# Tap products of blocks 1 and 2 summed by TensorE, halved weight low parts, and a new order of the opening

## Chip, cores and metric

The kernel runs on one core of one Trainium2 chip. The metric is device time in microseconds (us) from start to end of one execution, the median of several. An engine is named as the profile names it: PE is TensorE, DVE is VectorE, ACT is ScalarE, POOL is GpSimd, SP is SyncE, which issues most of the transfers.

## What is computed

A convolution whose taps come from the input, then two feed-forward layers, on 8192 tokens of 192 features (2 sequences of 4096):

```
w   = exp(weight_gen - max over 7 taps);  w = w / (sum over taps + 1e-9)          # 8 heads x 7 taps per token
x   = sum over k in 0..6 of w[:, k] * x_pad[token + k]                             # causal, one weight per head of 24 features
h   = x @ w_in                                                                     # 192 -> 2048
P   = a0 + a1 h + a2 h^2 + a3 h^3;   Q = 1 + |b0||h| + |b1| h^2;   g = P / (Q + 1e-6)
y   = g @ w_out                                                                    # 2048 -> 192
yn  = y / sqrt(mean(y^2) + 1e-6) * rms_g
out = (silu(yn @ w_gate) * (yn @ w_val)) @ w2_out                                  # 192 -> 1536 -> 192
```

## The kernel before

**Tiling.** The tokens are cut into 16 blocks of 512 (4 slots of 128). All weights stay in SBUF. Each product with w_in, w_gate and w_val is made of five matmuls on parts that are kept in a format with fewer bits: a high part, and a low part that holds the rest (`first_layer`). So each such weight has to be copied to its high part by ACT (`piece_high`) and its low part taken by a subtraction once at the start: pieces 0 to 3 (w_in) by DVE, pieces 4 to 7 (w_gate, w_val) by POOL, 128x1536 each (`piece_low`, L390). A piece is loaded into a buffer that is free at the start: piece 4 into `seed`, 5 and 6 into `stage`, 7 into `glu`.

**Stages of a block.** The 7 tap products and their 6 sums (rows by tokens); transposes of the sum on PE into two PSUM banks (`xpose`); high and low parts of the transposed x (`x_high` on ACT, `x_low` on DVE); 16 chunks of the first layer (`up1`, bank, five matmuls); for each chunk two ACT passes (`linear`) and three DVE passes (`horner`, L601, L602, L604, one operand in PSUM); per pair of chunks |Q| (`abs`), per four the reciprocal square root (`root`), its square (`square`), then on DVE `py` (L617), `qy` (L612) and `newton` (L623), all three with both operands in SBUF, 1024 columns; 16 `down1`; row norm (`ss`, `rms`, `xn`); its transposes (`xnx`), 12 `gate`, 12 `value`, `silu`, `glu` products, 12 `down2` into the banks of `dn2`, and the copy to the output (`y`).

**Order.** Each engine runs an order written out by hand (`PE_PROGRAM`, `ACT_PROGRAM`, `DVE_PROGRAM`, `POOL_PROGRAM`): entries are step, number and lag; in iteration i a step works on block i - lag. So iteration i of PE holds `up1` of block i-1, parts of `down1`, `gate` and `value` of block i-2, and `down2` of block i-3. In iterations 1 and 2 (written out, outside the loop) no block has come as far as `down2`. An engine takes its steps strictly in order; a step waits on semaphores for what it reads and for the buffer that it writes (`bank_read` with the table `BEFORE` for the four shared banks).

**Taps before.** Block 0: DVE makes the 7 products and 2 of the sums (`first_product`, `first_sum`) and PE flips and adds five tiles by matmuls with the identity that accumulate in the two banks of `xpose` (`flip_and_add`, L755 and L761). From block 1 on POOL makes 7 products (L409, L413) and 6 sums (L422, L424, L427), and PE only transposes the result (L693). Ahead of iteration 1 ACT does `exp`, the high parts of pieces 0 to 4 and then `x_high` of block 0; `root 0` of block 0 waits for the low part of piece 4, since it writes `seed`. SP issues block 0's rows, all eight pieces, w_out, and only then (after the last tap product of block 0) block 1's rows.

Of the kernel before, what the change touches and what calls it, by code (L numbers as in the profile page):

```python
# [129 lines left out]
def build(nc, x, weight_gen, w_in, w_out, a, b, w_gate, w_val, w2_out, rms_g, out):  # L130
# [17 lines left out]
    with ctx:  # L148
# [66 lines left out]
        tap0 = sem("tap0")  # L215
        sum0 = sem("sum0")
# [163 lines left out]
        def _(pool):  # L380
# [35 lines left out]
            def tap_add(blk, k):  # L416
                wait(pool, tap_ready, (blk - 1) * K + k + 1)
                if k > 1:
                    wait(pool, tap_sum, (blk - 1) * (K - 2) + k - 1)
# [3 lines left out]
                else:  # L423
                    pool.tensor_tensor(conv_twice, conv[:, :, DA:D], product[:, :, DA:D], ALU.add)\  # L424
                        .then_inc(twice_ready, 1)
                    wait(pool, twice_ready, blk)
                    pool.tensor_tensor(conv_rows, conv_rows, product, ALU.add).then_inc(conv_ready, 1)  # L427

            def rms_inverse(blk, _):
# [8 lines left out]
                                                "piece": piece_low}, LAST)  # L438

        @block.scalar  # L440
        def _(act):
# [42 lines left out]
            def root(blk, t):  # L484
# [172 lines left out]
        def _(pe):  # L657
# [4 lines left out]
            def bank_read(blk, name, n):  # L662

                i = blk + LAG[name, n]
                while True:
# [140 lines left out]
```

## Time and profile before

| | us |
|---|---|
| median of 3 runs | 1449.33 (1448.91 to 1449.6) |
| the profiled execution | 1448.36, of which the trace spans 1446.6 |
| busy in the span | PE 1381.6 (96%), DVE 1251.5 (87%), ACT 1070.6 (74%), POOL 461.6 (32%) |

The page cuts the span into 40 slices of 36 us; PE is at 9 tenths or more in all but the first four. Times below are us from the start of the span. In a row of the timeline the bracket is the idle time of the engine ahead of the instruction and what ended it. "PEclk" is the granted clock of PE as a share of its full speed: 1.0 is 2.4 GHz, 0.5 is 1.2 GHz.

### The profile page before, as it was taken

How to read it: one execution, taken by the hardware profiler on the slowest of the kernel's cores; microseconds unless marked ns; L12 is line 12 of the kernel's file. 1: busy time of each engine (PE TensorE's matmuls, PEld its weight loads, DVE VectorE, ACT ScalarE, POOL GpSimd, SP SyncE). 2: the span in 40 equal slices, each digit the busy share in tenths (PEclk: the TensorE clock that was granted, in tenths of full speed). 3: DMA queues.
4: the chain of work that ended last, by engine and by line, in shares of the span. 5: the costliest groups of instructions: out<-in, count | busy, mean ns of one | idle time of the engine just before them, and what ended most of it. 6: DMA issues, size and time to landing. Idle time of an engine off the chain costs nothing.

```text
span 1446.6 us, 20719 instructions
## 1 busy us (share of the span) xinstructions
PE 1381.6 (96%) x7192; PEld 1233.7 (85%) x7192; DVE 1251.5 (87%) x1519; ACT 1070.6 (74%) x1387; POOL 461.6 (32%) x283
## 2 busy tenths in 40 slices
PE   7566999999999999999999999999999999999999
PEld 6355889888898988889898888989888898988988
DVE  6999998989989898998989899898989989888621
ACT  4766877878887787878778787877878887777521
POOL 1846241434324143432414343142434314200000
PEclk9778999999999999999999999999999999999999
DMA  8200001000000100000010000001000000000000
GB/s 230 84 0 21 11 0 42 1 31 11 30 11 0 41 0 30 11 30 11 0 41 0 30 11 30 11 0 41 0 30 11 30 12 0 12 0 1 12 12 11
DMA packets 12515, 32.31 MB, mean 22 GB/s; under 512 B 1604, under 2 KB 7234, under 8 KB 12480
## 3 DMA queue, kind: packets, MB, share of 16 engines
q1 hardware_dynamic: 11744, 31.61, 6.8%
q8 instruction: 22, 0.36, 0.1%
q10 hardware_dynamic: 736, 0.23, 0.1%
q14 instruction: 13, 0.11, 0.0%
HBM read 25.55 MB, written 6.29 MB: 22 GB/s over the span
## 4 chain that ended last, share of the span: by engine, by line
PE 76%; DVE 11%; ACT 7%; issue 4%; DMA 1%; SPq 0%; ACTq 0%; POOL 0%; DVEq 0%; POOLq 0%
PE dn L686 32%; PE bank L677 9%; PE bank L678 8%; PE bank L679 8%; PE bank L680 8%; PE bank L681 8%; DVE den L612 4%; ACT seed L490 2%; PE bank L693 2%; DVE num L604 2%; DVE num L617 1%; DVE num L601 1%; DVE num L623 1%; ACT L490 1%; ACT seed L496 1%
## 5 line engine op out<-in xcount | busy, mean ns | idle before, releaser
L686 PE MATMUL dn<-dn_w,num 128*128 128x192 f32 x2048 | 380.2, 330 | 17.1 <-DVE num L623 10.0
L686 PEld LDWEIGHTS dn<-dn_w,num 128*128 128x128 f32 x2048 | 344.9, 193 | 24.2 <-DVE num L623 8.6
L475 ACT ACTIVATE den<-bank,coef 128x512 f32<-128x512 f32 x256 | 175.6, 686 | 180.6 <-PE bank L681 163.7
L686 PE MATMUL dn<-dn_w,glu 128*128 128x192 f32 x1536 | 280.9, 327 | 5.3 <-DVE glu L648 5.3
L686 PEld LDWEIGHTS dn<-dn_w,glu 128*128 128x128 f32 x1536 | 254.3, 190 | 13.2 <-DVE glu L648 9.2
L601 DVE TENSOR_TENSOR num<-num,bank 128x512 f32<-128x512 f32 x256 | 174.0, 680 | 65.3 <-ACT num L477 63.4
L617 DVE SCALAR_TENSOR_TENSOR num<-num,coef,seed 128x1024 f32<-128x1024 f32 x128 | 184.8, 1445 | 38.9 <-ACT seed L496 38.4
L477 ACT ACTIVATE num<-bank,coef 128x512 f32<-128x512 f32 x256 | 199.8, 781 | 0.0
L623 DVE SCALAR_TENSOR_TENSOR num<-den,num 128x1024 f32<-128x1024 f32 x128 | 194.5, 1521 | 0.0
L602 DVE SCALAR_TENSOR_TENSOR den<-den,coef,bank 128x512 f32<-128x512 f32 x256 | 189.1, 739 | 0.0
L604 DVE SCALAR_TENSOR_TENSOR num<-num,coef,bank 128x512 f32<-128x512 f32 x256 | 189.0, 738 | 0.0
L612 DVE SCALAR_TENSOR_TENSOR den<-den,seed 128x1024 f32<-128x1024 f32 x128 | 188.1, 1470 | 0.0
L648 DVE TENSOR_TENSOR glu<-glu,bank 128x512 f32<-128x512 f32 x192 | 130.5, 680 | 66.1 <-PE bank L681 64.8
L516 ACT ACTIVATE glu<-bank 128x512 f32<-128x512 f32 x192 | 113.2, 598 | 81.2 <-PE bank L681 76.2
L422 POOL TENSOR_TENSOR conv<-conv,prod 128x768 f32<-128x768 f32 x75 | 170.2, 2270 | 0.0
L677 PE MATMUL bank<-xn_ah,up_ah 128*128 128x512 f32 x384 | 163.0, 425 | 0.0
L482 ACT ACTIVATE den<-den 128x1024 f32<-128x1024 f32 x128 | 134.9, 1054 | 32.1 <-DVE num L604 32.1
L413 POOL TENSOR_TENSOR prod<-x_in,w_blk 128x768 f32<-128x768 f32 x84 | 154.5, 1846 | 4.4
L678 PE MATMUL bank<-xn_al,up_ah 128*128 128x512 f32 x384 | 150.1, 391 | 0.0
L679 PE MATMUL bank<-xn_ah,up_al 128*128 128x512 f32 x384 | 149.9, 390 | 0.0
L680 PE MATMUL bank<-xn_b,up_bh 128*128 128x512 f32 x384 | 149.7, 390 | 0.0
L681 PE MATMUL bank<-xn_b,up_bl 128*128 128x512 f32 x384 | 149.5, 389 | 0.0
(106 smaller groups left out, 2004.5 us busy)
## 6 DMA issues: line engine op xcount, KB each, us to landing
x_in<-in_x_dram SPq DMA_DIRECT2D x14, 960.0 KB
out_dram<-y_out SPq DMA_DIRECT2D x16, 384.0 KB, 2.3
w_blk<-in_weight_gen_dram SPq DMA_DIRECT2D x14, 112.0 KB, 2.0
dn_w<-in_moe_w_out_dram SPq DMA_DIRECT2D x1, 1536.0 KB, 21.0
dn_w<-in_moe_w_out_dram SPq DMA_DIRECT2D x1, 1152.0 KB, 10.2
num<-in_moe_w_in_dram SPq DMA_DIRECT2D x1, 768.0 KB, 6.1
num<-in_moe_w_in_dram SPq DMA_DIRECT2D x2, 384.0 KB, 7.8
seed<-in_moe_w_gate_dram SPq DMA_DIRECT2D x1, 768.0 KB, 10.2
```

The source lines that it names most:

```text
L477: act.activation(chunk(num, c), h, ACT.Identity, scale=na(3), bias=na(2)).then_inc(lin_ready, 1)
L602: dve.scalar_tensor_tensor(d, d, B_ABS[:, 0:1], h, ALU.add, ALU.mult)
L604: dve.scalar_tensor_tensor(n, n, na(1), h, ALU.add, ALU.mult).then_inc(poly_ready, 1)
L612: dve.scalar_tensor_tensor(d, d, EPS_Q, y, ALU.add, ALU.mult).then_inc(qy_ready, 1)
L617: dve.scalar_tensor_tensor(n, n, na(0), y, ALU.add, ALU.mult).then_inc(py_ready, 1)
L623: dve.scalar_tensor_tensor(n, d, -2.0, n, ALU.add, ALU.mult).then_inc(act_ready, 1)
L677: pe.matmul(out_bank[:, :], ah, m_ah[:, :], start=True, stop=False)
L678: pe.matmul(out_bank[:, :], ah, m_al[:, :], start=False, stop=False)
L679: pe.matmul(out_bank[:, :], al, m_ah[:, :], start=False, stop=False)
L680: pe.matmul(out_bank[:, :], bh, m_b[:, :], start=False, stop=False)
L681: return pe.matmul(out_bank[:, :], bl, m_b[:, :], start=False, stop=True)
L686: done = pe.matmul(banks[:, j // 2, j % 2 * D:(j % 2 + 1) * D], acts[:, j * P:(j + 1) * P], w, start=first and j % 2 == 0, stop=last, skip ...
```

## The change

Iteration 1 holds the front of block 0 and the taps of block 1; iteration 2 those of blocks 1 and 2.

- For blocks 1 and 2 POOL makes the 7 products only, each into one of four tiles in turn. PE flips each product and adds it up in the two banks of `dn2`, which hold nothing before iteration 3 (steps `tap1` and `tap2`, placed in PE's order behind named `up1` and `down1` steps). The sums on POOL and the transposes of these blocks go. A product that reuses a tile waits until PE has flipped what was in it (`flipped`).
- The low parts of pieces 4 to 7 are taken in halves of 768 columns, eight instructions, each behind a DVE count (`LOW_BEHIND`); the products of block 2 are placed in the same way (`MUL_BEHIND`).
- Opening: ACT copies x of block 0 ahead of the high parts of pieces 3 and 4; pieces 4 to 7 go behind `abs 3`, `root 1`, `linear 9` and `abs 4`. SP loads block 1's rows ahead of w_out and of pieces 4 to 7. Piece 4 is staged in the buffer of `xn_t` and `square` in place of `seed`. DVE makes three of block 0's sums, PE flips four tiles.
- The rest follows from these (counts of semaphores that start at block 3, three guarding waits).

```diff
-down1 10 2, down2 1 3, down1 11 2, down2 2 3, value 3 3, gate 5 3, up1 4 1, value 4 3, up1 5 1, down1 12 2,
-down2 3 3, down1 13 2, value 5 3, up1 6 1, gate 6 3, up1 7 1, down2 4 3, down1 14 2, down2 5 3, down1 15 2,
-value 6 3, gate 7 3, value 7 3, gate 8 3, up1 8 1, up1 9 1, gate 9 3, up1 10 1, down2 6 3, down1 0 1,
+down1 10 2, down2 1 3, down1 11 2, down2 2 3, value 3 3, gate 5 3, up1 4 1, tap1 0 0, value 4 3, up1 5 1,
+tap1 1 0, down1 12 2, down2 3 3, down1 13 2, value 5 3, up1 6 1, tap1 2 0, tap2 0 0, gate 6 3, up1 7 1, tap1 3 0,
+tap2 1 0, down2 4 3, down1 14 2, down2 5 3, down1 15 2,
+value 6 3, gate 7 3, value 7 3, gate 8 3, up1 8 1, tap1 4 0, tap2 2 0, up1 9 1, tap1 5 0, tap2 3 0, gate 9 3,
+up1 10 1, tap1 6 0, tap2 4 0, down2 6 3, down1 0 1,
...
-down1 1 1, xnx 0 2, down2 9 3, down1 2 1, xnx 1 2, down1 3 1, up1 12 1, up1 13 1, up1 14 1, up1 15 1,
+down1 1 1, xnx 0 2, down2 9 3, down1 2 1, xnx 1 2, down1 3 1, tap2 5 0, up1 12 1, up1 13 1, tap2 6 0, up1 14 1, up1 15 1,
...
-silu 6 3, abs 2 1, linear 7 1, piece 5 1, ss 0 2, silu 7 3, abs 3 1, piece 6 1, silu 8 3, root 1 1, piece 7 1, linear 8 1, linear 9 1,
-linear 10 1, square 2 1, silu 9 3, abs 4 1, silu 10 3, linear 11 1, silu 11 3, square 3 1, xn_high 0 2,
+silu 6 3, abs 2 1, linear 7 1, ss 0 2, silu 7 3, abs 3 1, piece 4 1, silu 8 3, root 1 1, piece 5 1, linear 8 1, linear 9 1,
+piece 6 1, linear 10 1, square 2 1, silu 9 3, abs 4 1, piece 7 1, silu 10 3, linear 11 1, silu 11 3, square 3 1, xn_high 0 2,
...
-add 6 1, piece 5 2, piece 6 2, piece 7 2, less 0 0, norm 0 0, mul 0 0, mul 1 0, mul 2 0, add 1 0, mul 3 0, add 2 0, mul 4 0, rms 0 2, add 3 0,
-mul 5 0, add 4 0, mul 6 0, add 5 0,
+add 6 1, low 4 2, low 5 2, low 6 2, low 7 2, less 0 0, norm 0 0, mul 0 0, mul 1 0, mul 2 0, add 1 0, mul 3 0, add 2 0, mul 4 0, rms 0 2, add 3 0,
+mul 5 0, add 4 0, mul 6 0, add 5 0, low 0 1, low 1 1, low 2 1, low 3 1,
...
+ALONE = {"tap1": 1, "tap2": 2}
+FLIPPED_IN_SUMS = (0, 1, 2)
...
-              "mul": 1, "add": 1, "xpose": 1, "x_high": 1, "x_low": 1}
+              "mul": 1, "add": 3, "xpose": 3, "x_high": 1, "x_low": 1}
...
+            elif name in ALONE:
+                there = isinstance(i, int) and i - lag == ALONE[name]
...
-        xn_t = sb("xn_t", [P, SLOTS, D + DB])
+        norm_rows = sb("norm_rows", [P, SLOTS * (D + DB) + ROW])
+        xn_t = norm_rows[:, 0:SLOTS * (D + DB)].rearrange("p (j d) -> p j d", j=SLOTS)
+        square = norm_rows[:, SLOTS * (D + DB):].rearrange("p (j d) -> p j d", j=SLOTS)
...
-            ([w_gate[0:DA, :]], seed[:, 0:F2], up2_ah[:, 0, :], up2_al[:, 0, :]),
+            ([w_gate[0:DA, :]], norm_rows[:, 0:F2], up2_ah[:, 0, :], up2_al[:, 0, :]),
...
-        LOWS = len(PIECES) - BY_DVE
+        LOWS = 2 * (len(PIECES) - BY_DVE)
...
+        TILES = [slots(prod[:, 0, :]), slots(prod[:, 1, :]), conv_rows, y_out[:, :, :]]
+
+        def tile(blk, k):
+            return TILES[((blk - 1) * K + k) % len(TILES)]
...
+        def x_bank(blk, part):
+
+            if isinstance(blk, int) and blk in (1, 2):
+                return dn2[:, part, :]
+            return bank[XPOSE_BANK[part]][:, :]
...
-            for n in range(len(PIECES)):
+            for n in range(BY_DVE):
                 load_piece(n)
+            sp.wait_ge(tap0, K)
+            load_first(1)
             src, dst = DOWN[0]
             sp.dma_start(dst[:, :, :], src).then_inc(down_in[0], 16)
-            sp.wait_ge(tap0, K)
-            load_first(1)
             sp.dma_start(w_blk[:, :], w_rows[:, 2 * SLOTS * HK:3 * SLOTS * HK]).then_inc(wgen_in, 16)
+            sp.wait_ge(xt_ready, 2)
+            for n in range(BY_DVE, len(PIECES)):
+                load_piece(n)
             src, dst = DOWN[1]
             sp.dma_start(dst[:, :, :], src).then_inc(down_in[1], 16)
...
-            def piece_low(_, n):
-                pool.wait_ge(whi, n + 1)
-                pool.tensor_tensor(PIECES[n][3], PIECES[n][1], PIECES[n][2], ALU.subtract).then_inc(wlo, 1)
...
+            LOW_BEHIND = [(act_ready, 2)] * 3 + [(qy_ready, 3), (py_ready, 4)] + [(act_ready, 4)] * 3
+            MUL_BEHIND = [(qy_ready, 7)] * 3 + [(py_ready, 8)] * 2 + [(qy_ready, 9)] * 2
+
+            def half_low(_, n):
+                piece = BY_DVE + n // 2
+                cols = slice(n % 2 * F2 // 2, (n % 2 + 1) * F2 // 2)
+                pool.wait_ge(whi, piece + 1)
+                pool.wait_ge(*LOW_BEHIND[n])
+                pool.tensor_tensor(PIECES[piece][3][:, cols], PIECES[piece][1][:, cols], PIECES[piece][2][:, cols],
+                                   ALU.subtract).then_inc(wlo, 1)
...
-            pool.wait_ge(wlo0, BY_DVE)
-            piece_low(0, BY_DVE)
+
+            def early_product(blk, k):
+
+                turn = (blk - 1) * K + k - len(TILES)
+                if turn < 0:
+                    pool.wait_ge(xt_ready, 2)
+                elif turn % K == K - 1:
+                    pool.wait_ge(xt_ready, 2 * (turn // K + 2))
+                else:
+                    pool.wait_ge(flipped, turn // K * (K - 1) + turn % K + 1)
+                if k == 0:
+                    pool.wait_ge(x_in_ready, x_count(blk))
+                    pool.wait_ge(sm_norm, soft_count(blk))
+                if blk == 2:
+                    pool.wait_ge(*MUL_BEHIND[k])
+                pool.tensor_tensor(by_slot(tile(blk, k)), slot_heads(rows_of(k)), slot_heads(taps_of(k, blk)), ALU.mult)\
+                    .then_inc(tap_ready, 1)
...
-                if k == 0:
+                if isinstance(blk, int) and blk in FLIPPED_IN_SUMS:
+                    early_product(blk, k)
...
             exponentials(0, 0)
-            for n in range(5):
+            for n in range(3):
                 piece_high(0, n)
             x_high(0, 0)
             x_high(0, 1)
+            piece_high(0, 3)
...
-                if isinstance(blk, int) and (blk, t) == (0, 0):
-                    act.wait_ge(wlo, 1)
...
+                if isinstance(blk, int) and blk == 0:
+                    act.wait_ge(wlo, 2)
...
+                if isinstance(blk, int) and blk == 0:
+                    act.wait_ge(xt_ready, 6)
...
+                    dve.wait_ge(sum0, 2)
...
-            for k in range(5):
+            first_product(0)
+            for k in (1, 3, 5):
                 first_product(k)
-            first_sum(3)
-            for k in range(5, K):
-                first_product(k)
-            first_sum(5)
+                first_product(k + 1)
+                first_sum(k)
             for n in range(2):
...
+                        pe.wait_ge(x_ready, 6)
...
-            def flip_and_add(tile, first, last):
+            def flip_and_add(blk, rows, first, last):
                 for j in range(SLOTS):
-                    done = pe.matmul(bank[XPOSE_BANK[0]][:, j * P:(j + 1) * P], tile[:, j, 0:DA], ident[:, :],
+                    done = pe.matmul(x_bank(blk, 0)[:, j * P:(j + 1) * P], rows[:, j, 0:DA], ident[:, :],
                                      start=first and j == 0, stop=last, skip_group_check=True)
                 if last:
                     done.then_inc(xt_ready, 1)
                 for j in range(SLOTS):
                     for half in range(0, P, DB):
-                        done = pe.matmul(bank[XPOSE_BANK[1]][half:half + DB, j * P:(j + 1) * P], tile[:, j, DA:D], ident[:, :],
+                        done = pe.matmul(x_bank(blk, 1)[half:half + DB, j * P:(j + 1) * P], rows[:, j, DA:D], ident[:, :],
                                          start=first and j == 0, stop=last, skip_group_check=True)
                 if last:
                     done.then_inc(xt_ready, 1)
+                elif blk > 0:
+                    done.then_inc(flipped, 1)
+
+            def early_tap(blk, k):
+                pe.wait_ge(tap_ready, (blk - 1) * K + k + 1)
+                if (blk, k) == (2, 0):
+                    pe.wait_ge(x_ready, 4)
+                flip_and_add(blk, tile(blk, k), k == 0, k == K - 1)
             pe.wait_ge(consts, 3)
             for n in range(WARM):
                 pe.matmul(bank[XPOSE_BANK[0]][:, 0:P], ident[:, :], ident[:, :], start=True, stop=True)
-            for k in (0, 1, 2):
-                pe.wait_ge(tap0, k + 1)
-                flip_and_add(FIRST[k], k == 0, False)
-            pe.wait_ge(sum0, 1)
-            flip_and_add(FIRST[3], False, False)
-            pe.wait_ge(sum0, 2)
-            flip_and_add(FIRST[5], False, True)
+            pe.wait_ge(tap0, 1)
```

## Rows read from the trace of the kernel before

**Rows 1.** Stretches: length; busy PE, PEld, DVE, ACT, POOL; PEclk, DMA share, GB/s.

```profile
70.00:80.00 10.00, 3.82 (x11) 3.07 (x12) 10.00 (x6) 2.36 (x4) 10.00 (x3) 0.66 0.00 0
...
200.00:400.00 200.00, 199.10 (x1040) 178.22 (x1039) 181.51 (x223) 157.99 (x211) 73.17 (x45) 1.00 0.06 21
```

**Rows 2.** Chain that ended last, in order of time: start, length, what.

```profile
12.71 10.24 DMA seed<-in_moe_w_gate_dram
22.97 1.48 ACT up_ah L457
...
25.76 0.71 DVE x_b L576
26.56 0.76 PE bank L677
```

**Rows 3.** Timeline, block 0's flips on PE (start, us, engine, line, what).

```profile
18.86 1.16 PE L755 MATMUL bank<-ident,xn_t 128*128 128x128 f32 x8
19.95 1.09 PE L761 MATMUL bank<-ident,xn_t 128*64 128x128 f32 x16
```

**Rows 4.** Groups of DVE's instructions from 43 to 83 us: busy, mean ns.

```profile
L612 DVE SCALAR_TENSOR_TENSOR den<-den,seed 128x1024 f32<-128x1024 f32 x4 | 13.9, 3478 | 0.0
L623 DVE SCALAR_TENSOR_TENSOR num<-den,num 128x1024 f32<-128x1024 f32 x3 | 7.9, 2653 | 0.0
L617 DVE SCALAR_TENSOR_TENSOR num<-num,coef,seed 128x1024 f32<-128x1024 f32 x4 | 7.6, 1922 | 1.7 <-ACT seed L496 1.7
```

**Rows 5.** Timeline of DVE, opening and iterations 1 and 2.

```profile
9.39 1.83 DVE L564 TENSOR_TENSOR prod<-x_in,w_first 128x768 f32<-128x768 f32 x2 [0.68 <-DMA x_in<-in_x_dram]
...
43.95 4.94 DVE L617 SCALAR_TENSOR_TENSOR num<-num,coef,seed 128x1024 f32<-128x1024 f32 x2 [1.70 <-ACT seed L496]
...
74.13 0.68 DVE L601 TENSOR_TENSOR num<-num,bank 128x512 f32<-128x512 f32 x1
...
76.05 2.56 DVE L623 SCALAR_TENSOR_TENSOR num<-den,num 128x1024 f32<-128x1024 f32 x1
...
82.96 1.27 DVE L617 SCALAR_TENSOR_TENSOR num<-num,coef,seed 128x1024 f32<-128x1024 f32 x1
...
117.44 1.21 DVE L612 SCALAR_TENSOR_TENSOR den<-den,seed 128x1024 f32<-128x1024 f32 x1
```

**Rows 6.** Groups of DVE's instructions from 83.1 to 154.1 us.

```profile
L623 DVE SCALAR_TENSOR_TENSOR num<-den,num 128x1024 f32<-128x1024 f32 x8 | 13.4, 1690 | 0.0
L617 DVE SCALAR_TENSOR_TENSOR num<-num,coef,seed 128x1024 f32<-128x1024 f32 x9 | 12.1, 1352 | 0.7 <-ACT seed L496 0.7
L612 DVE SCALAR_TENSOR_TENSOR den<-den,seed 128x1024 f32<-128x1024 f32 x8 | 12.0, 1510 | 0.0
```

**Rows 7.** Timeline of POOL.

```profile
30.00 3.51 POOL L390 TENSOR_TENSOR up_al<-seed,up_ah 128x1536 fp32r<-128x1536 f32 x1 [12.97 <-DVE up_bl L550]
40.51 1.55 POOL L409 TENSOR_TENSOR conv<-x_in,w_first 128x768 f32<-128x768 f32 x1 [7.00 <-DMA x_in<-in_x_dram]
...
77.49 4.46 POOL L390 TENSOR_TENSOR up_bl<-glu,up_bh 128x1536 fp32r<-128x1536 f32 x1
```

**Rows 8.** Timeline of ACT.

```profile
57.63 2.00 ACT L490 ACTIVATE seed<-den,coef 128x2048 f32<-128x2048 f32 x1
...
60.91 0.67 ACT L475 ACTIVATE den<-bank,coef 128x512 f32<-128x512 f32 x1
...
62.14 0.69 ACT L475 ACTIVATE den<-bank,coef 128x512 f32<-128x512 f32 x1
```

**Rows 9.** Timeline of PE: a wait in iteration 2, and `up1 14`.

```profile
117.58 5.49 PE L686 MATMUL dn<-dn_w,num 128*128 128x192 f32 x16 [4.46 <-DVE num L623]
...
154.94 0.50 PE L677 MATMUL bank<-x_ah,up_ah 128*128 128x512 f32 x1 [2.33 <-DVE xn_al L639]
```

**Rows 10.** Busy time by stretch, iteration 2, and one stretch at half clock.

```profile
103.60:154.90 51.30, 35.03 (x156) 29.87 (x154) 50.60 (x55) 35.58 (x52) 27.62 (x16) 0.87 0.07 22
117.50:123.00 5.50, 5.42 (x17) 5.42 (x18) 5.50 (x9) 5.35 (x6) 0.00 (x0) 0.50 0.00 0
```

More of the change, by code:

```diff
@@ L93 @@
 STORE_LAG = 2
-ONCE = ("piece",)
+ONCE = ("piece", "low")
+ALONE = {"tap1": 1, "tap2": 2}
+FLIPPED_IN_SUMS = (0, 1, 2)
 FROM_BLOCK = {"peak": 2, "less": 2, "exp": 2, "inverse": 2, "norm": 2,
-              "mul": 1, "add": 1, "xpose": 1, "x_high": 1, "x_low": 1}
+              "mul": 1, "add": 3, "xpose": 3, "x_high": 1, "x_low": 1}
 LAG = {(name, n): lag for name, n, lag in PE_PROGRAM}
 def run_iterations(eng, order, ops, last):
-    trail = max(lag for _, _, lag in order)
+    trail = max(3, max(lag for _, _, lag in order))
     def iteration(i):
@@ L215, in build @@
         tap0 = sem("tap0")
+        flipped = sem("flipped")
         sum0 = sem("sum0")
@@ L399, in _ @@
             pool.memset(x_in[:, 0:(HALO - SLOTS) * D], 0.0).then_inc(halo0, 1)
-            pool.wait_ge(wlo0, BY_DVE)
-            piece_low(0, BY_DVE)
+            def early_product(blk, k):
[13 more added lines that the diff above has]
+                    .then_inc(tap_ready, 1)
             def tap_product(blk, k):
-                if k == 0:
+                if isinstance(blk, int) and blk in FLIPPED_IN_SUMS:
+                    early_product(blk, k)
+                elif k == 0:
                     wait(pool, x_in_ready, x_count(blk))
@@ L411, in tap_product @@
                     if k >= 3:
-                        wait(pool, tap_sum, (blk - 1) * (K - 2) + k - 2)
+                        wait(pool, tap_sum, (blk - 3) * (K - 2) + k - 2)
                     pool.tensor_tensor(by_head(prod[:, k % 2, :]), rows_of(k), taps_of(k, blk), ALU.mult)\
@@ L418, in tap_add @@
                 if k > 1:
-                    wait(pool, tap_sum, (blk - 1) * (K - 2) + k - 1)
+                    wait(pool, tap_sum, (blk - 3) * (K - 2) + k - 1)
                 product = slots(prod[:, k % 2, :])
@@ L425, in tap_add @@
                         .then_inc(twice_ready, 1)
-                    wait(pool, twice_ready, blk)
+                    wait(pool, twice_ready, blk - 2)
                     pool.tensor_tensor(conv_rows, conv_rows, product, ALU.add).then_inc(conv_ready, 1)
@@ L437, in _ @@
                                                 "less": peak_taken_off, "norm": normalised_taps,
-                                                "piece": piece_low}, LAST)
+                                                "low": half_low}, LAST)
         @block.scalar
@@ L461, in x_high @@
                 wait(act, xt_ready, blk * 2 + (part + 1))
-                act.activation((x_ah, x_b)[part][:, :], bank[XPOSE_BANK[part]][:, :], ACT.Copy).then_inc(xt_hi, 1)
+                act.activation((x_ah, x_b)[part][:, :], x_bank(blk, part), ACT.Copy).then_inc(xt_hi, 1)
             exponentials(0, 0)
-            for n in range(5):
+            for n in range(3):
                 piece_high(0, n)
@@ L562, in first_product @@
                 elif k == 6:
-                    dve.wait_ge(sum0, 1)
+                    dve.wait_ge(sum0, 2)
                 dve.tensor_tensor(by_slot(FIRST[k]), slot_heads(rows_of(k)), slot_heads(taps_of(k, 0)), ALU.mult)\
@@ L573, in x_low @@
                 if part == 0:
-                    dve.tensor_tensor(x_al[:, :], bank[XPOSE_BANK[0]][:, :], x_ah[:, :], ALU.subtract).then_inc(x_ready, 1)
+                    dve.tensor_tensor(x_al[:, :], x_bank(blk, 0), x_ah[:, :], ALU.subtract).then_inc(x_ready, 1)
                 else:
-                    dve.tensor_tensor(x_b[DB:P, :], bank[XPOSE_BANK[1]][DB:P, :], x_b[DB:P, :], ALU.subtract)\
+                    dve.tensor_tensor(x_b[DB:P, :], x_bank(blk, 1)[DB:P, :], x_b[DB:P, :], ALU.subtract)\
                        .then_inc(x_ready, 1)
-            for k in range(5):
+            first_product(0)
+            for k in (1, 3, 5):
                 first_product(k)
-            first_sum(3)
-            for k in range(5, K):
-                first_product(k)
-            first_sum(5)
+                first_product(k + 1)
+                first_sum(k)
             for n in range(2):
@@ L668, in bank_read @@
                     blk = i - LAG[name, n]
-                    if not isinstance(blk, int) or 0 <= blk <= LAST or i < 0:
+                    if not isinstance(blk, int) or i < 0:
+                        break
+                    if 0 <= blk <= LAST and not (name == "xpose" and blk in (1, 2)):
                         break
@@ L696, in transposes @@
             def transposes(blk, part):
-                wait(pe, conv_ready, blk)
+                wait(pe, conv_ready, blk - 2)
                 bank_read(blk, "xpose", part)
@@ L768, in _ @@
                 pe.matmul(bank[XPOSE_BANK[0]][:, 0:P], ident[:, :], ident[:, :], start=True, stop=True)
-            for k in (0, 1, 2):
-                pe.wait_ge(tap0, k + 1)
-                flip_and_add(FIRST[k], k == 0, False)
-            pe.wait_ge(sum0, 1)
-            flip_and_add(FIRST[3], False, False)
-            pe.wait_ge(sum0, 2)
-            flip_and_add(FIRST[5], False, True)
+            pe.wait_ge(tap0, 1)
+            flip_and_add(0, FIRST[0], True, False)
+            for k in (1, 3, 5):
+                pe.wait_ge(sum0, (k + 1) // 2)
+                flip_and_add(0, FIRST[k], False, k == 5)
             pe.wait_ge(wlo0, 2)
@@ L779, in _ @@
                 "up1": up1, "down1": down1, "gate": gate, "value": value, "down2": down2,
-                "xnx": xn_transposes, "xpose": transposes}, LAST)
+                "xnx": xn_transposes, "xpose": transposes, "tap1": early_tap, "tap2": early_tap}, LAST)
 _INS = ['x', 'weight_gen', 'moe_w_in', 'moe_w_out', 'moe_a', 'moe_b',
```

1 line of the change is left out of this document (removed).

## Prediction

> **What bounds the kernel now.** The share of busy time names PE, but the stretches show two regimes. From 200 us on PE is busy 199.1 of 200 us at full clock [rows 1]: what is left there is a fixed amount of PE's work, and the change doesn't touch it. From about 26 to 155 us it is otherwise: between 70 and 80 us DVE and POOL are busy 10.0 of 10 us and PE 3.8 [rows 1]. The time is therefore set by how soon PE gets into its steady run. I date that by `up1 14` of block 1 at 154.94, PE's last wait ahead of it (2.33 us, for `xn_low` on DVE) [rows 9]; earlier by x, the whole is shorter by x.
>
> DVE's groups say why the opening is long. Before 83 us its passes with both operands in SBUF take 3.48, 2.65 and 1.92 us (L612, L623, L617) [rows 4], where the same passes take 1.21 and 1.27 us with POOL quiet [rows 5]. Passes with an operand in PSUM aren't stretched: a chunk's three passes ran from 74.13 to 76.05, 1.92 us, in a stretch in which POOL was never idle [rows 1, 5]. Against 1.21 (L612, L623) and 1.27 (L617) the excess up to 83 us is 13.9-4.8 + 7.9-3.6 + 7.6-5.1 = 15.9 us [rows 4]; after it 13.4-9.7 + 12.1-11.4 + 12.0-9.7 = 6.7 us [rows 6]. Together 22.6 us of DVE's path are owed to POOL.
>
> **1. The opening: 4.3 us.** The chain is x of block 0 [rows 2]: ACT's copy of x stood behind the high part of piece 4 (22.97 + 1.48), which waited for its load; the first matmul came at 26.56. Now the copy waits for the flips alone. DVE starts at 9.39 and makes one sum more: ten passes of 0.9 us [rows 5] end at 18.5; PE flips one tile less. A set is 18.86 to 21.04, 2.1 us start to start [rows 3]; the last set starts at 18.6 and ends at 20.8. Then ACT's copy of the second half (0.6 after 20.9), DVE's part of 0.71 and 0.1 to the matmul [rows 2]: 22.3. Gain 26.56 - 22.3 = 4.3. Piece 3's parts, now behind the copy, are ready at about 25.6, and `up1 4` needs them at 29. The 0.8 us that ACT, DVE and PE leave each other here is all known; bounds 3.5 to 4.6.
>
> **2. Iteration 1: 9.9 us.** Block 1's rows are issued at 17.5 and not behind six other transfers. They landed at 40.5 [rows 7]. Nothing shows their new time; piece 4, of the same size and also behind 2 MB, took 10.24 us [rows 2], so 27.7 at the latest and 17.5 as a floor. POOL's first product (1.55 us [rows 7]) is then ready by 29.3; PE asks for it at 30.2, behind `up1 4` (22.3 plus the 7.9 us that its first five `up1` took). Cover 0.9 us.
>
> PE has room for the seven sets (3.8 us busy of 10 at 70 us [rows 1]), but two stand in ACT's way. The first comes between `up1 4` and `up1 5` and holds `linear 5`, `abs 1` and `root 0` back by 0.7 us: `py 0`, at 43.95 before [rows 5], starts at 43.95 - 4.3 + 0.7 = 40.3. From there to `py 3` (82.96) DVE took 39.0 us, 23.1 without the excess of 15.9. Now the pieces' low parts wait until DVE reads PSUM. A half is 1.75 (half of 3.51) to 2.2 us (half of 4.46) [rows 7]; three of them (5.3 us) lie beside three chunks (5.8 us), the others beside one chunk each. Six of the products are over before 40 us; the seventh waits for the third set, at 39.4, and meets `py 0`: 0.8 us, between 0 and its whole 1.55.
>
> **A new wait** eats part of this. Once `newton` isn't stretched, ACT is late: behind `qy 1` come `root 1` (2.0 us), piece 5 (1.45 as in [rows 2]) and `linear 8` (1.23) [rows 8] before DVE may start `horner 8`. By hand along the queues: `qy 1` ends 49.65, but ACT is in piece 4 until 51.05; root until 53.05, piece until 54.5, linear until 55.75. DVE is through both newtons at 51.95: it idles 3.8 us. Pieces 6 and 7 delay `linear 10` and `11` for another 0.65 in sum. So 23.1 + 0.8 + 3.8 + 0.7 = 28.4 in place of 39.0, and `py 3` starts at 68.75, earlier by 14.2 (4.3 - 0.7 + 10.6; the 9.9 above).
>
> **3. Iteration 2: 3.5 us.** Up to `horner 0` of block 1 (102.6) POOL was quiet in both; the 14.2 stands. The products of block 2 now wait for `qy 6`, which gives back the 2.0 us that `py 6` and `qy 6` lost: 16.2. From here PE is the tighter queue. From 103.6 to 154.9 it was busy 35.0 of 51.3 us at a mean clock of 0.87; in 117.5 to 123.0 it ran at 1.2 GHz (0.50) after a wait of 4.46 us [rows 9, 10]. Without that stretch (2.7 us) and two shorter ones (1.6) its work is 30.7; seven sets of 2.1 make 45.4 us, and DVE needs 51.3 - 6.7 = 44.6 for its own. Two queues of 45 us that wait on each other don't both run full. By hand: waits of 2.5 us before `down1 12` (for `newton 6`) and 1.7 before `up1 6`; product 4 waits for a set that PE makes only behind `up1 6`, so it meets `newton 7` or `py 0`, and products 5 and 6, behind `rms`, meet `qy 1` and the newtons: 3.1 us for the three, between 0 and 3 x 1.55 = 4.7. `xn_low` then ends at 137.0 and PE reaches `up1 14` at 137.2: 154.9 - 137.2 = 17.7 us earlier. Four transposes go as well, but at that point PE and DVE are level, so I count nothing for them (up to 1 us).
>
> The other waits cost nothing: `y` of block 0 for the flips of block 2, `ss` for piece 4's low part and the first `down2` for `x_low` of block 2 all ask for what `up1 0` of block 2 or an earlier step had to have. SP's later pieces are wanted from 49.6 us on, 9 us after the whole load had ended before (the rows of block 1, behind w_out, landed at 40.5 [rows 7]).
>
> **Sum.** 4.3 + 9.9 + 3.5 = 17.7 us. Against the profiled execution, 1448.36 - 17.7 = 1430.7; the median of the runs lies 0.97 above that execution: 1431.6, and I give 1431.5.
>
> **A rule against the price of a meeting.** My 0.8 and 3.1 us let DVE and POOL both crawl on: two `py` took 4.94 where 2.5 are usual [rows 5]. The Trainium skill (SBUF — State Buffer, Who interferes with whom) says that the pair of ports is an exclusive lock: who comes first keeps it for the whole instruction. By it each of the four meetings costs DVE a product's whole length, 6.2 us in place of 3.9. This is in the second rival, and what hangs on the rule alone is 2.3 us.
>
> **Rivals.**
> *More of it (10%):* ACT gives nothing back, since pieces 4 and 5 lie better than by hand, and nothing meets: 3.8 + 0.7 less in iteration 1, of which PE passes on some 3 us: 21 us, 1427 to 1428. For it: the 22.6 are real. Against it: the order of ACT's steps is fixed and its durations are known.
> *More given back (28%):* meetings at the full length (+2.3), two or three PE waits of over 4 us that bring 1.2 GHz again (2.7 each [rows 10]), or rows of block 1 landing late by 2 us. Gain 9 to 14: 1435 to 1440. For it: in iteration 2 the loop product, set, tile, product is closed over three engines.
> *Not at all what it says (3%):* rows of block 1 still land at 40.5. Then PE waits for the first product behind `up1 4` until 42.1, `py 0` slips 12 us and the gain is 2 to 8 us: 1441 to 1447.
> *Slower (6%):* the sets don't fill gaps but stand in series. Each holds the next `up1`, so `linear`, `horner` and the product that asks for the tile. In series they cost 14 x 2.1 = 29.7, with ACT's 4.5 and the meetings' 3.9 38.1, against 22.6 + 4.3 = 26.9 saved: 11 us slower, 1460. It decides from about nine of the 14 sets in series (18.5 us). Against it: PE idled 6.2 of 10 us at 70 us and 16.3 of 51.3 later [rows 1, 10], and by hand one set of the first seven holds anybody up. A mild form, ten to eleven sets, gives 1451 to 1454.
>
> **How the numbers follow.** My forecast of 1431.5 with its own range of 1428 to 1435 has 53%. The range for 8 in 10 leaves out the slower case, the late rows and the tails of the others: 1426 to 1440. A measurement of this kernel tells about 0.2% (2.9 us) from no change. Faster by more: 53 + 10 + 28 and most of the 3, 0.92; within 0.2%: 0.03; slower by more: 0.05.
>
> **What would show each step.** Step 1: the first L677 at 22.3. Step 2: a DVE wait of about 3.8 us ahead of L601 for ACT's L477 near 52 us, `py 3` near 68.8, L612 at a mean near 1.3 before it, POOL's halves at 1.8 us. Step 3: PE busy over 90% from 89 us on, `up1 14` near 137. I am wrong if PE waits for POOL's products, if L612 and L623 still stretch beyond 1.6 us in the mean, or if after 140 us PE, now 18 us ahead, waits for DVE again.

## The result and the profile after

Four runs of the changed kernel gave a median of 1429.13 us (1427.42 to 1430.10) against 1449.12 of before (four runs, 1448.85 to 1449.60): 20.0 us less, ratio 0.986 with a 95% interval of 0.9843 to 0.9878. The profiled execution, the slowest of the four, took 1430.10, its trace spans 1428.3 us.

Busy time by stretch of the changed kernel (length; busy PE, PEld, DVE, ACT, POOL with their instructions; granted clock, DMA share, GB/s):

```profile
29.90:33.70 3.80, 3.80 (x27) 3.31 (x25) 3.80 (x7) 2.31 (x3) 1.19 (x1) 0.56 1.04 244
46.00:105.00 59.00, 45.06 (x241) 38.91 (x237) 54.16 (x71) 46.60 (x55) 22.57 (x14) 0.86 0.00 1
105.20:138.00 32.80, 32.74 (x264) 28.89 (x264) 32.74 (x41) 24.52 (x37) 8.96 (x5) 1.00 0.10 34
...
200.00:400.00 200.00, 199.10 (x1051) 178.95 (x1050) 179.86 (x225) 156.99 (x203) 63.37 (x40) 1.00 0.07 23
```

The last row is as before [rows 1]; the third is new: from 105.2 us on PE doesn't wait, where before it was busy 35.0 of 51.3 us [rows 10]. The groups of DVE from 43 to 69 us, which answer to [rows 4]:

```profile
L668 DVE SCALAR_TENSOR_TENSOR num<-num,coef,seed 128x1024 f32<-128x1024 f32 x4 | 5.0, 1281 | 3.4 <-ACT seed L544 3.4
L663 DVE SCALAR_TENSOR_TENSOR den<-den,seed 128x1024 f32<-128x1024 f32 x4 | 4.9, 1219 | 0.0
...
L652 DVE TENSOR_TENSOR num<-num,bank 128x512 f32<-128x512 f32 x6 | 4.1, 684 | 3.8 <-ACT num L527 3.8
L674 DVE SCALAR_TENSOR_TENSOR num<-den,num 128x1024 f32<-128x1024 f32 x3 | 3.6, 1220 | 0.0
```

`qy` (L663) takes 1.22 us in the mean where it took 3.48. In exchange DVE now waits 3.8 us in sum for ACT's `linear` (L527), 3.60 of them at 56.35. The dates of DVE on its path, from its timeline:

```profile
21.18 0.69 DVE L628 TENSOR_TENSOR x_b<-bank,x_b 64x512 fp32r<-64x512 f32 x1 [0.27 <-ACT x_b L511]
...
23.58 3.10 DVE L602 TENSOR_TENSOR up_bl<-num,up_bh 128x1536 fp32r<-128x1536 f32 x1
...
41.90 2.48 DVE L668 SCALAR_TENSOR_TENSOR num<-num,coef,seed 128x1024 f32<-128x1024 f32 x2 [3.35 <-ACT seed L544]
...
56.35 0.69 DVE L652 TENSOR_TENSOR num<-num,bank 128x512 f32<-128x512 f32 x1 [3.60 <-ACT num L527]
...
68.93 1.28 DVE L668 SCALAR_TENSOR_TENSOR num<-num,coef,seed 128x1024 f32<-128x1024 f32 x1
...
108.17 3.77 DVE L668 SCALAR_TENSOR_TENSOR num<-num,coef,seed 128x1024 f32<-128x1024 f32 x2
...
117.96 2.35 DVE L674 SCALAR_TENSOR_TENSOR num<-den,num 128x1024 f32<-128x1024 f32 x2
```

And of PE, with the first `up1`, the first two sets of flips and `up1 14` of block 1 (the last row):

```profile
21.98 0.47 PE L730 MATMUL bank<-x_ah,up_ah 128*128 128x512 f32 x1 [1.47 <-DVE x_b L628]
...
28.87 0.47 PE L730 MATMUL bank<-x_ah,up_ah 128*128 128x512 f32 x1 [2.07 <-DVE num L655]
...
30.32 1.91 PE L809 MATMUL dn<-ident,prod 128*128 128x128 f32 x8
32.16 1.59 PE L815 MATMUL dn<-ident,prod 128*64 128x128 f32 x16
...
34.96 1.05 PE L809 MATMUL dn<-ident,prod 128*128 128x128 f32 x8
35.94 1.09 PE L815 MATMUL dn<-ident,prod 128*64 128x128 f32 x16
...
66.79 0.79 PE L730 MATMUL bank<-x_ah,up_ah 128*128 128x512 f32 x1 [4.99 <-DVE num L655]
...
105.26 0.50 PE L730 MATMUL bank<-x_ah,up_ah 128*128 128x512 f32 x1 [1.38 <-DVE num L655]
...
138.02 0.50 PE L730 MATMUL bank<-x_ah,up_ah 128*128 128x512 f32 x1
```

`up1 14` came at 154.94 [rows 9] and comes at 138.02, 16.9 us earlier; the rest of the span shrank from 1291.7 to 1290.3 us. 16.9 + 1.4 = 18.3 us, the difference of the two spans.

### The profile page after: what moved, and what is told of

Same layout as the page of the kernel before. It is cut to its first block, busy times and chain, and to the rows that moved or that the text cites. A ratio compares the mean times of both kernels' runs of the same rounds, so it can differ in the third digit from the quotient of the medians.

```text
span 1428.3 us, 21289 instructions
## 1 busy us (share of the span) xinstructions
PE 1396.2 (98%) x7488; PEld 1249.2 (87%) x7488; DVE 1231.4 (86%) x1520; ACT 1070.5 (75%) x1387; POOL 430.9 (30%) x273
## 4 chain that ended last, share of the span: by engine, by line
PE 80%; DVE 8%; ACT 7%; issue 4%; DMA 0%; ACTq 0%; DVEq 0%
PE dn L739 34%; PE bank L730 9%; PE bank L731 9%; PE bank L732 9%; PE bank L734 9%; PE bank L733 9%; DVE den L663 3%; ACT seed L538 2%; PE bank L746 2%; ACT L538 1%; DVE num L655 1%; ACT seed L544 1%; ACT L502 1%; DVE num L652 1%; ACT num L527 1%
## 5 line engine op out<-in xcount | busy, mean ns | idle before, releaser
L739 PE MATMUL dn<-dn_w,num 128*128 128x192 f32 x2048 | 375.6, 328 | 4.0 <-DVE num L674 4.0
L739 PEld LDWEIGHTS dn<-dn_w,num 128*128 128x128 f32 x2048 | 340.9, 191 | 10.7 <-DVE num L674 5.2
L668 DVE SCALAR_TENSOR_TENSOR num<-num,coef,seed 128x1024 f32<-128x1024 f32 x128 | 181.7, 1421 | 43.0 <-ACT seed L544 42.5
L527 ACT ACTIVATE num<-bank,coef 128x512 f32<-128x512 f32 x256 | 199.9, 781 | 0.0
L674 DVE SCALAR_TENSOR_TENSOR num<-den,num 128x1024 f32<-128x1024 f32 x128 | 186.7, 1460 | 0.0
L663 DVE SCALAR_TENSOR_TENSOR den<-den,seed 128x1024 f32<-128x1024 f32 x128 | 176.9, 1383 | 0.0
L532 ACT ACTIVATE den<-den 128x1024 f32<-128x1024 f32 x128 | 134.9, 1055 | 19.3 <-DVE num L655 19.3
L471 POOL TENSOR_TENSOR conv<-conv,prod 128x768 f32<-128x768 f32 x65 | 147.2, 2264 | 0.0
L462 POOL TENSOR_TENSOR prod<-x_in,w_blk 128x768 f32<-128x768 f32 x78 | 142.5, 1834 | 4.1
```

What stands on the lines that cost most here:

```text
L527: act.activation(chunk(num, c), h, ACT.Identity, scale=na(3), bias=na(2)).then_inc(lin_ready, 1)
L663: dve.scalar_tensor_tensor(d, d, EPS_Q, y, ALU.add, ALU.mult).then_inc(qy_ready, 1)
L674: dve.scalar_tensor_tensor(n, d, -2.0, n, ALU.add, ALU.mult).then_inc(act_ready, 1)
L739: done = pe.matmul(banks[:, j // 2, j % 2 * D:(j % 2 + 1) * D], acts[:, j * P:(j + 1) * P], w, start=first and j % 2 == 0, stop=last, skip ...
```

## The experiments

Three groups of kernels, each beside runs of the kernel before of its own. "Gain" is the median of those minus the median of the kernel; the changed kernel has 20.0 and, run again in the second group, 20.2 us (ratio 0.9857, 0.9842 to 0.9872). A difference of two kernels under some 1 us isn't told apart by these runs. Below, a pass of DVE *meets* an instruction of POOL when the two run at once and the pass has both operands in SBUF, and its *excess* is what it takes beyond the 1.21 or 1.27 us (1.75 for a low part) that it takes with POOL quiet.

### The opening alone

```diff
 # before.py
-            for n in range(5):
+            for n in range(3):
                 piece_high(0, n)
             x_high(0, 0)
             x_high(0, 1)
+            piece_high(0, 3)
+            piece_high(0, 4)
...
 # and three first_sums on DVE, four flips on PE, as in the change
```

> The kernel before with one part of the change: ACT copies x of block 0 ahead of the high parts of pieces 3 and 4, DVE makes three sums, PE flips four tiles. SP's order, POOL's work and the staging stay. If the opening's 4.6 us (first up1 at 26.56 before, 21.98 after) is passed on whole to the end, 4.3 to 4.6 us less than before: 1444.6. If it is eaten later, because POOL's lows and sums meet DVE in other places, the gain is under 2 us.

Gain 10.0 us (1439.01 against 1448.98; ratio 0.9935, 0.9916 to 0.9954). Both readings were wrong: it gives twice what it takes off the opening. DVE's groups from 36 to 156 us, first of the kernel before, then of this one:

```profile
L612 DVE SCALAR_TENSOR_TENSOR den<-den,seed 128x1024 f32<-128x1024 f32 x12 | 25.9, 2166 | 0.0
L623 DVE SCALAR_TENSOR_TENSOR num<-den,num 128x1024 f32<-128x1024 f32 x11 | 21.3, 1953 | 0.0
L617 DVE SCALAR_TENSOR_TENSOR num<-num,coef,seed 128x1024 f32<-128x1024 f32 x12 | 18.4, 1549 | 2.4 <-ACT seed L496 2.4
```

```profile
L624 DVE SCALAR_TENSOR_TENSOR num<-den,num 128x1024 f32<-128x1024 f32 x12 | 22.5, 1890 | 0.0
L613 DVE SCALAR_TENSOR_TENSOR den<-den,seed 128x1024 f32<-128x1024 f32 x12 | 20.9, 1749 | 0.0
L618 DVE SCALAR_TENSOR_TENSOR num<-num,coef,seed 128x1024 f32<-128x1024 f32 x13 | 19.5, 1510 | 2.5 <-ACT seed L498 2.4
```

Against 1.21 and 1.27 us undisturbed [rows 5] the excess is 11.4 + 8.0 + 3.2 = 22.6 us before and 8.0 + 6.4 + 3.0 = 17.4 here. `py 0` starts at 38.61 (43.95 before), 5.3 us earlier; 5.3 + 5.2 = 10.5. POOL's work is the same, and its products still start at 40.3, when block 1's rows land; moved by 5 us against it, DVE's passes meet less of it (17.4 against 22.6). Nothing else of their work differs, so which passes are met is a matter of phase, and the parts of this change don't add up.

### Sums back on POOL

```diff
 # after.py
-FLIPPED_IN_SUMS = (0, 1, 2)
+FLIPPED_IN_SUMS = (0,)
-ALONE = {"tap1": 1, "tap2": 2}
+ALONE = {"tap1": -1, "tap2": -1}
-              "mul": 1, "add": 3, "xpose": 3, "x_high": 1, "x_low": 1}
+              "mul": 1, "add": 1, "xpose": 1, "x_high": 1, "x_low": 1}
...
 # the counts of tap_sum, twice_ready and conv_ready as before, x in the two shared banks
```

> The changed kernel with products and sums of blocks 1 and 2 back on POOL and transposes on PE; opening, placed halves of the low parts and ACT's order stay. Theory: sums on POOL meet DVE's passes in SBUF again, about 3 us in iteration 1 and the 6.7 us of before in iteration 2, less 2 us since no set of flips holds linear 5: 6 to 8 us slower than the changed kernel, 12 to 14 us faster than before, so 1435 to 1437. Rival, that the flips carry nearly the whole gain: 1443 or more. Rival, that PE's added work costs what POOL's sums cost: within 3 us of the changed kernel.

Gain 10.4 us (1438.56), 9.6 less than the changed kernel; I had expected 6 to 8 less. In the same window:

```profile
L661 DVE SCALAR_TENSOR_TENSOR den<-den,seed 128x1024 f32<-128x1024 f32 x12 | 20.1, 1680 | 0.0
L672 DVE SCALAR_TENSOR_TENSOR num<-den,num 128x1024 f32<-128x1024 f32 x12 | 18.6, 1566 | 0.0
L666 DVE SCALAR_TENSOR_TENSOR num<-num,coef,seed 128x1024 f32<-128x1024 f32 x12 | 18.6, 1559 | 2.4 <-ACT seed L542 2.4
```

The excess is 5.6 + 4.1 + 3.4 = 13.1 us; in the changed kernel it is 1.3 (one pair of `py`). `py 0` is 4.2 us earlier than before, the excess 9.5 us smaller, and DVE waits 3.6 us for ACT as in the changed kernel: 4.2 + 9.5 - 3.6 = 10.1. So the placed halves and the early rows alone add nothing to the opening alone, for what they save DVE idles behind ACT. I had too small an excess for iteration 1: 3 us, where the pair of `py` (5.20 us), two `qy` (2.82 and 2.85) and a `newton` (1.63) give some 6.4. The sums on PE are worth about 10 us on top (1.4 of them are the two transposes of block 2, which stand behind `up1 14`: from there on this kernel needs 1291.7 us like the one before, the changed kernel 1290.3); the rival of "PE's work costs what POOL's sums cost" is out.

### The low parts not placed; the products not placed

```diff
 # after.py
-                pool.wait_ge(*LOW_BEHIND[n])
```

> The changed kernel without the waits that place the eight half low parts behind counts of DVE; they start as soon as their high part is there. Theory: they then meet newton 1, py 2, qy 2 and newton 2 and cost DVE 2 to 4 us: 1431 to 1433. Rival, that ACT's order alone spaces them: within 1 us of the changed kernel.

Gain 17.3 us (1431.72; ratio 0.9875, 0.9858 to 0.9891): 2.7 to 2.9 less than the changed kernel, as expected. `py 2` and `qy 2` met halves:

```profile
59.84 2.34 DVE L667 SCALAR_TENSOR_TENSOR num<-num,coef,seed 128x1024 f32<-128x1024 f32 x1
62.10 2.82 DVE L662 SCALAR_TENSOR_TENSOR den<-den,seed 128x1024 f32<-128x1024 f32 x1
```

1.1 + 1.6 = 2.7 us of excess. Its profiled execution is the fastest of its four runs, as fast as the profiled one of the changed kernel (1429.94 and 1430.10): another meeting didn't happen in it, which is used below, and `py 0` started at 38.69 for 41.90. The 2.7 us are seen in the path and in the medians, not in these two times.

```diff
 # after.py
-                if blk == 2:
-                    pool.wait_ge(*MUL_BEHIND[k])
```

> The changed kernel without the waits that place block 2's products; they start when the normalised taps are there and a tile is free. Theory: products 1 and 2 meet py 6 and qy 6 of block 0, 1.5 to 2.5 us for DVE, and down1 12 waits for it: 1430.5 to 1431.5. Rival, that PE, the tighter queue in iteration 2, hides it: within 0.7 us of the changed kernel.

Gain 18.7 us (1430.32; ratio 0.9869, 0.9849 to 0.9889). The difference of 1.3 to 1.5 us isn't safe, the intervals overlap; the trace shows the expected meeting, `py 6` at 2.01 and `qy 6` at 2.56 us, 2.1 of excess (1.28 and 1.22 in the changed kernel).

### ACT's order, PE's order

```diff
 # after.py, ACT_PROGRAM
-silu 6 3, abs 2 1, linear 7 1, ss 0 2, silu 7 3, abs 3 1, piece 4 1, silu 8 3, root 1 1, piece 5 1, linear 8 1, linear 9 1,
+silu 6 3, abs 2 1, linear 7 1, piece 4 1, piece 5 1, ss 0 2, silu 7 3, abs 3 1, silu 8 3, root 1 1, linear 8 1, linear 9 1,
```

> The changed kernel with pieces 4 and 5 on ACT ahead of abs 3, in the 3.1 us in which ACT waits for horner 7, in place of ahead of and behind root 1. Theory: DVE's new wait ahead of horner 8 (3.60 us) is owed to these two copies; it falls to about 0.8 us and the whole is 2.5 to 2.9 us shorter: 1426.4. Rival, that PE or the loads set this stretch: within 0.7 us of the changed kernel.

Gain 22.8 us (1426.48 against 1449.31; ratio 0.9841, 0.9827 to 0.9854), 2.7 us (1426.48 against 1429.15) on top of the changed kernel run beside it. DVE's wait:

```profile
52.86 0.69 DVE L652 TENSOR_TENSOR num<-num,bank 128x512 f32<-128x512 f32 x1 [1.09 <-ACT num L527]
```

1.09 in place of 3.60 us: 2.5 us of the new wait were owed to the two copies, and they stood on the path. The profiled execution gained 1.0 us more ahead of this wait, from PE's clock (last section), which may be in the 2.7 in part.

```diff
 # after.py, PE_PROGRAM
-up1 4 1, tap1 0 0, value 4 3, up1 5 1,
-tap1 1 0, down1 12 2,
+up1 4 1, value 4 3, up1 5 1,
+tap1 0 0, tap1 1 0, down1 12 2,
```

> The changed kernel with the first set of flips behind up1 5, not ahead of it. Theory: linear 5 starts 2.3 us sooner, root 0 and py 0 2.0 us sooner; product 6 now meets py 0 and takes up to 1.5 of it: 0.5 to 2 us shorter, 1427.6. Rival, that horner 4 and 5 and not linear 5 release root 0: no difference.

Gain 20.7 us, 0.5 more than the changed kernel: not told apart. The trace shows both halves of the expectation:

```profile
39.67 3.69 DVE L668 SCALAR_TENSOR_TENSOR num<-num,coef,seed 128x1024 f32<-128x1024 f32 x2 [1.71 <-ACT seed L544]
```

`py 0` starts at 39.67 and not after 41, but the pair now meets product 6 and takes 3.69 for 2.48.

> Both moves. If their gains add up: 3.2 to 4.7 us shorter than the changed kernel, 1425. If one hides the other: no more than the better of the two.

Both edits at once: gain 22.8 us (1426.46), the same as the first alone. What the second brings forward, product 6 takes again (the pair of `py` takes 3.77 for 2.48).

### PE's room

```diff
 # after.py; zeros is a 128x128 tile of zeros
             def early_tap(blk, k):
...
+                if blk == 2 and k:                     # blk == 1 in the second kernel
+                    flip_and_add(blk, tile(blk, k), False, False, zeros)
                 flip_and_add(blk, tile(blk, k), k == 0, k == K - 1)
```

> The changed kernel with six more sets of 24 matmuls on PE in iteration 2: ahead of sets 1 to 6 of block 2 the same tile is multiplied by zeros and added to the same banks. Six sets of 2.05 us are 12.3 us. Theory: from up1 6 of block 1 (105.3) to up1 14 (138.0) PE doesn't wait, so all of it lands on the end, 11 to 12.5 us slower than the changed kernel: 1441. Rival, that DVE sets the end of iteration 2 and PE has room there: 0 to 4 us slower.

Gain 6.8 us (1442.14 against 1448.90): 13.2 to 13.4 slower than the changed kernel for 12.3 us of added work. In iteration 2 PE has no room at all; DVE now waits for `linear` behind late `up1` steps, 3.4 us the longest.

> The changed kernel with six more sets on PE in iteration 1, made in the same way ahead of sets 1 to 6 of block 1: 12.3 us of PE's work. Theory: PE waits 0.6 and 5.0 us there, and linear 6 to 10 lie 3 to 7 us behind their up1, so more than half is hidden: 3 to 6 us slower than the changed kernel, 1433.5. Rival, that sets stand in series with the chain of up1, linear and horner: 12 us slower, 1441.

Gain 17.0 us (1431.93): 3.0 to 3.2 slower for the same work. By the medians three quarters of it are hidden. The profiled execution says somewhat less: no meeting delayed it ahead of `py 0` (38.75 for 41.90), and from there to `up1 14` it took 5.0 us more than the changed kernel (101.1 for 96.1), so that three fifths are hidden. Either way the sets of block 1 stand in series with nothing for most of their length. The rival that ended slower than before needed nine of 14 sets in series; the sets of block 1 aren't.

### All meetings placed

Both moves of ACT and PE, and

```diff
 # after.py
+                if (blk, k) == (1, 0):
+                    pool.wait_ge(wlo0, BY_DVE)
+                if (blk, k) == (1, 6):
+                    pool.wait_ge(qy_ready, 1)
-            MUL_BEHIND = [(qy_ready, 7)] * 3 + [(py_ready, 8)] * 2 + [(qy_ready, 9)] * 2
+            MUL_BEHIND = [(qy_ready, 7)] * 3 + [(py_ready, 8)] + [(qy_ready, 9)] * 3
```

> Pieces 4 and 5 ahead of abs 3 and set 0 behind up1 5, and three more products placed: the first one of block 1 waits for DVE's last low part, the last one of block 1 for qy 0, product 4 of block 2 for qy 0 of block 1. Theory: a product that starts ahead of a DVE pass costs it 1.3 us; without the first two py 0 and qy 0 are over 2.6 us sooner than with the two moves alone, the third is hidden by PE: 5 to 5.5 us less than the changed kernel, 1424. Rival, that DVE's gain ends in a wait of its own, as with the two moves together: 1426.5, no better than pieces 4 and 5 moved alone.

Median 1423.73 us (1423.50 to 1424.01), gain 25.2 us, ratio 0.9825 (0.9812 to 0.9839): 5.0 us more than the changed kernel run in the second group. Its DVE starts `py 0` over 3 us earlier, and no pass is stretched before the sums of block 3 begin on POOL (L667 at 154.31, 2.56 us):

```profile
38.34 2.48 DVE L672 SCALAR_TENSOR_TENSOR num<-num,coef,seed 128x1024 f32<-128x1024 f32 x2 [1.71 <-ACT seed L548]
...
101.70 2.48 DVE L672 SCALAR_TENSOR_TENSOR num<-num,coef,seed 128x1024 f32<-128x1024 f32 x2
```

Of the 5.0 us, 2.6 come with the two moves (gain 22.8 against 20.2). The other 2.4 agree with two meetings of iteration 1 that are gone: the last low part takes 1.75 us for 3.10 and the pair of `py` 2.48 for 3.77, 2.6 together. The third meeting went too (the second row), and gave nothing: from `py 3` to `up1 14` it is 68.7 us here and 68.8 with both moves, for here too PE works without a gap once `up1 6` has started (98.8 to 131.5: 32.70 of 32.70 us busy). The five runs lie within 0.5 us, those of the changed kernel within 2.7 and, run again, 1.5. That fits a meeting and a clock that fall one way or the other from run to run (below), but wasn't tried by itself.

## Why the prediction was right, and where not

The forecast was 1431.5, the measured median 1429.1.

**The bound** was read rightly: the opening set the time, DVE set the opening, POOL stretched DVE. The excess of 22.6 us fell to 1.3; another 1.3 arose ahead of that window, in DVE's last low part.

**Step 1.** First matmul forecast at 22.3, measured 21.98: 4.6 us in place of 4.3. What I missed is what it does later: alone it is worth 10.0 us, since it shifts DVE against POOL. In the whole change this can't be added, for there the meetings go anyway.

**Step 2.** `py 3` forecast at 68.75, measured 68.93, but that is luck in part: a start 1.6 us late and a path 1.4 us shorter cancelled. The rows of block 1 had landed by 23.35 (I had 17.5 to 27.7), well ahead of PE's need, and so early that product 0 met DVE's last low part, which took 3.10 us for the 1.76 of the one before it. Then the first set of flips ran at 1.2 GHz, 3.4 us in place of 2.1: PE had waited 2.07 us for `horner 0`, and the granted clock of 29.9 to 33.7 was 0.56. `py 0` started at 41.90 where I had 40.3. On the other side DVE took 27.0 us from there to `py 3` and not 28.4: product 6 was over by 41.94 and met nothing (I had 0.8), and the waits for ACT were some 0.6 shorter in sum. The new wait for ACT, forecast 3.8, was 3.60, and the run with the pieces moved shows what the two copies in it cost: some 2.5.

**Step 3.** `up1 14` forecast at 137.2, measured 138.0. Inside it two sizes were off, again in opposite directions. I gave the products of block 2 3.1 us of DVE's time; they took 1.3, product 4 alone (3.77 for the pair of `py` at 108.17), and even these didn't reach the end, as the last experiment shows. Products 5 and 6 took nothing from `qy 1` and the newtons (2.35 the pair). And DVE and PE weren't level: `xn_low` began at 134.9 and PE came 3.1 us later; its last wait was 1.38 us ahead of 105.26, and six more sets cost more than their length. So from there PE was the bound of iteration 2, and the transposes that I counted at nothing ("up to 1 us") did show: 1.4 us less behind `up1 14`, which the kernel with the sums back on POOL loses again.

**The sum** was 17.7 us; the profiled execution shows 18.3, the medians 20.0. The last 1.7 us are the place of the profiled executions: that of the changed kernel lies 1.0 above its median, that of the kernel before 0.8 below. The forecast had no term for that.

**The rivals.** *More of it* comes near in time (1427 to 1428), but not by its mechanism: ACT did give 3.60 us back. *More given back* named the right dangers, meetings and clock. Two passes lost 1.3 us each, and PE's clock cost the first set of flips 1.3. It fell again behind PE's one wait of over 4 us (4.99 at 66.79; 0.50 from 66.8 to 70.4) and behind waits of 3.16 and 2.46 us (0.52 from 80.7 to 91.0), where I had 2.7 us for each fall. DVE, which had the path there, shows next to nothing of it: its waits up to 105 us are 0.68 us at 91.27, as long as before the change, and 0.19 at 95.91. *Slower* fell with the doubled sets; its sum has a slip (14 x 2.1 is 29.4, not 29.7), which changes nothing. *Late rows* fell with the first product at 23.35.

**The rule on the ports.** I had priced a meeting at 0.8 to 1.0 us and set the Trainium skill's rule (SBUF — State Buffer, Who interferes with whom) of an exclusive lock held for the whole instruction against it. The same pass in two kernels decides: in the changed kernel product 0 started at 23.35, ahead of the low part at 23.58, and DVE took 3.10 us. In the kernel with low parts not placed the order was the other way:

```profile
23.31 1.75 DVE L601 TENSOR_TENSOR up_bl<-num,up_bh 128x1536 fp32r<-128x1536 f32 x1
...
23.54 2.93 POOL L446 TENSOR_TENSOR prod<-x_in,w_first 128x768 f32<-128x768 f32 x1 [6.06 <-issue]
```

DVE's 1.75 us are undisturbed and the product takes 2.93 for its 1.54: it waited for the 1.5 us that DVE had left. By that rule, the trace agrees: of the two that overlap the second waits until the first is through. (Product 0 itself took 1.72 us in the changed kernel, for it started while the low part before, 21.91 to 23.67, was still running.) Which of the two comes first is open from run to run: DVE's low part took 3.10 us in eight of the ten profiled executions in which product 0 isn't placed, and 1.75 in two. Of my four meetings one happened, at 1.3 us; the other 1.3 us belong to this one, which I hadn't counted.

## What to carry to other kernels

Where two engines stretch each other, list who starts first in each meeting: moving the slack engine's instruction behind one count of the tight engine turned a 1.3 us cost into none, and three such waits with two moves in the order brought 5 us here, half of it by the waits. A stretched engine hides its suppliers' lateness; before counting the whole excess as gain, walk the supplier's queue (here ACT's, which took 3.6 us of the gain). Work moved to an engine with idle time is cheap only in the stretch that has the idle time: the same 12.3 us cost 3 to 5 in one iteration and 13 in the next.

## What the runs showed of the hardware that I had not expected

A product on POOL that meets a series of DVE passes in SBUF can wait for the whole series, not only for the pass in hand. In the changed kernel the two products at 117.62 lie beside `qy 1` (from 116.83) and both newtons (to 120.3); of this tile:

```profile
L447 POOL TENSOR_TENSOR prod<-x_in,w_blk x2: 1542/2820/4098, 117.6 to 121.7; 128x768 f32<-128x768 f32 x2
```

The first took 4.10 us and ended at 121.7, 1.5 us after DVE's last pass of the series, the second its usual 1.54. In the kernel with all meetings placed the small `rms` of POOL shows the same: 2.74 us for its usual 0.19, from 109.87 to behind both newtons (110.19 to 112.55), and DVE then waited 1.20 us for it. At 108.69 of the changed kernel, though, a product got in between two `py` passes: it took 2.16 and DVE's pair 3.77. What decides between the two isn't shown by these runs.

PE's clock fell after a wait of 2.07 us in the changed kernel's profiled execution (0.56 in 29.9 to 33.7), and after 2.08 us when that kernel was run again (0.65). In the kernel with pieces ahead of `abs 3`, with the same work up to there and a wait of 2.11 us, it didn't:

```profile
29.90:33.70 3.80, 3.80 (x36) 3.28 (x35) 3.80 (x7) 2.73 (x4) 2.44 (x2) 1.00 1.05 262
```

Of eight profiled executions of the changed kernel and its variants with a wait of 2.07 to 2.11 us there, three show the clock fallen (0.56, 0.65 and 0.65) and five don't (1.00). In the three in which the last low part met nothing the wait was 0.72 to 0.76 us, and the clock stayed at 1.00. So this one meeting seems to cost twice, once on DVE and, in some executions, once more on PE behind the wait that it makes; what decides whether the clock falls isn't shown.

In the kernel with pieces ahead of `abs 3` product 4, which waits for the first set, then started at 31.97 and not at 33.85, and `py 0` at 40.02; there it met product 6, and the pair of `py` took 3.38, which gives back half of what was gained:

```profile
31.97 1.55 POOL L447 TENSOR_TENSOR prod<-x_in,w_first 128x768 f32<-128x768 f32 x1 [1.18 <-PE dn L815]
...
40.02 3.38 DVE L668 SCALAR_TENSOR_TENSOR num<-num,coef,seed 128x1024 f32<-128x1024 f32 x2 [2.02 <-ACT seed L544]
```
